# Attention and two feed-forward layers in one kernel: rows of x as dm = 96r + 32k + p, and the state updated head by head in 64-column tiles

## What is computed

```python
B, H, S, D = q.shape                      # 4, 8, 768, 48
f = 1.0 / (1.0 + np.exp(-f_logit))
for t in range(S):
    state = f[:, :, t, :, None] * state + np.einsum('bhd,bhe->bhde', k[:, :, t], v[:, :, t])
    y[:, :, t] = np.einsum('bhd,bhde->bhe', q[:, :, t], state)
x = y.transpose(0, 2, 1, 3).reshape(B * S, H * D)       # 3072 x 384
h = x @ w_in; x2 = (h * sigmoid(1.702 * h)) @ w_out     # 384 -> 2048 -> 384
p = probs / (probs.sum(-1) + 1e-9)
out = sum(p[:, e] * (relu(x2 @ w1[e]) @ w2[e]) for e in range(4))   # 384 -> 1024 -> 384
```

## Time and profile before

| | us |
|---|---|
| median of 3 runs (1355.3 to 1356.3) | 1356.08 |
| the profiled execution | 1355.08 |
| its span, first to last instruction | 1353.3 |
| PE busy | 1326.8 |
| DVE, POOL, ACT busy | 890.9, 629.0, 568.4 |
| half 0 alone | about 0 to 60 |
| seven rounds | about 60 to 536 |
| the rest | 536 to 1353 |

### The profile page before, as it was taken

The page is one execution under the profiler, slowest core; times in us unless marked ns, Lnnn a source line. Parts: engine busy times, 40 slices in busy tenths (PEclk is TensorE's granted clock), DMA queues, the critical chain, the costliest instruction groups (busy, mean ns, idle before and its releaser), DMA issues.

```text
span 1353.3 us, 26477 instructions
## 1 busy us (share of the span) xinstructions
PE 1326.8 (98%) x10837; PEld 1233.1 (91%) x10837; DVE 890.9 (66%) x1354; ACT 568.4 (42%) x975; POOL 629.0 (46%) x721
## 2 busy tenths in 40 slices
PE   6899999999999999999999999999999999999999
PEld 5788999999999999998999999999999999999998
DVE  8786858475858583566666666666666666666666
ACT  5673636363636363453233333333323433334341
POOL 8786747484747573655121212112212544443330
PEclk9999999999999999999999999999999999999999
DMA  9636252525252521220101101010001112222211
GB/s 157 135 74 104 60 84 63 86 61 85 62 88 59 87 59 40 79 74 24 35 13 35 36 13 35 12 36 24 25 24 59 36 47 70 71 70 75 66 35 47
DMA packets 240200, 79.34 MB, mean 59 GB/s; under 512 B 189136, under 2 KB 238544, under 8 KB 240080
## 3 DMA queue, kind: packets, MB, share of 16 engines
q1 hardware_dynamic: 201680, 74.11, 23.0%
q10 hardware_dynamic: 38400, 3.55, 2.2%
HBM read 67.83 MB, written 9.78 MB: 57 GB/s over the span
## 4 chain that ended last, share of the span: by engine, by line
PE 89%; ACT 3%; DVE 2%; issue 2%; POOL 2%; SPq 1%; DMA 1%; ACTq 0%; DVEq 0%; POOLq 0%
PE bank L1917 10%; PE bank L1915 10%; PE bank L1916 10%; PE bank L1851 9%; PE bank L1852 9%; PE bank L1850 9%; PE bank L1823 5%; PE bank L1582 4%; PE bank L1825 4%; PE bank L1824 4%; PE bank L1580 4%; PE bank L1581 4%; PE bank L1635 3%; PE bank L1591 1%; PE bank L1781 1%
## 5 line engine op out<-in xcount | busy, mean ns | idle before, releaser
L1529 DVE SCALAR_TENSOR_TENSOR acc<-bank,p_n,acc 128x384 f32<-128x384 f32 x384 | 235.0, 612 | 67.9 <-PE bank L1917 62.9
L1917 PE MATMUL bank<-w_h,h_l 128*128 128x384 f32 x768 | 257.3, 335 | 0.0
L1915 PE MATMUL bank<-w_h,h_h 128*128 128x384 f32 x768 | 257.2, 335 | 0.0
L1916 PE MATMUL bank<-w_l,h_h 128*128 128x384 f32 x768 | 257.0, 335 | 0.0
L1513 DVE TENSOR_TENSOR bank<-bank,x_copy 128x512 f32<-128x512 f32 x192 | 124.5, 694 | 165.9 <-ACT x_copy L1187 102.4
L836 POOL TENSOR_TENSOR g_l<-sig,g_h 128x384 fp32r<-128x384 f32 x128 | 157.7, 1232 | 157.4 <-ACT g_h L1090 157.3
L1852 PE MATMUL bank<-xs,we_l 128*128 128x512 f32 x528 | 206.5, 391 | 0.0
L1851 PE MATMUL bank<-xs,we_h 128*128 128x512 f32 x528 | 206.4, 391 | 0.0
L1850 PE MATMUL bank<-xs,we_h 128*128 128x512 f32 x528 | 205.5, 389 | 0.7 <-issue 0.7
L888 POOL TENSOR_TENSOR we_l<-we_raw,we_h 128x384 fp32r<-128x384 f32 x96 | 96.5, 1033 | 215.4 <-ACT we_h L1155 215.3
L1187 ACT ACTIVATE x_copy<-bank 128x512 f32<-128x512 f32 x144 | 86.1, 598 | 222.1 <-PE bank L1852 221.7
(11 more groups left out here) (156 smaller groups left out, 2387.2 us busy)
## 6 DMA issues: line engine op xcount, KB each, us to landing
we_raw<-in_moe_w SPq DMA_DIRECT2D x32, 384.0 KB, 3.9
w_raw<-in_moe_w SPq DMA_DIRECT2D x32, 384.0 KB, 3.3
v_sb<-in_v SPq DMA_DIRECT2D x48, 96.0 KB, 2.7
x_dram<-work SPq DMA_DIRECT2D x8, 576.0 KB, 4.7
x_raw<-x_dram SPq DMA_DIRECT2D x12, 384.0 KB, 4.4
f_raw<-in_f_logit SPq DMA_DIRECT2D x56, 72.0 KB, 2.1
q_raw<-in_q SPq DMA_DIRECT2D x56, 72.0 KB, 2.0
k_raw<-in_k SPq DMA_DIRECT2D x56, 72.0 KB, 2.1
```

The lines of the kernel that those rows point to most:

```text
L1529: dve.scalar_tensor_tensor(acc[:, pr * TT + i, :], y_bank[y % 3][:, 0:DM], p_n[:, col:col + 1], acc[:, pr * TT + i, :], ALU.mult, ALU.add) ...
L1915: pe.matmul(dst, hh, wh, start=f == 0, stop=False)
L1916: pe.matmul(dst, hh, wl, start=False, stop=False)
L1917: last = pe.matmul(dst, hl, wh, start=False, stop=f == 1)
```

## The change

x's rows in the three chunks of 128 become dm = 96r + 32k + p. v is laid out with 64 columns a head (48 and 16 zeros), and tile k of pair r takes 32 columns that stand side by side: k = 0 lies in the first head, k = 2 in the second, and k = 1 has 16 columns of each with zeros beside them, so it needs two products and the others one. `state_columns`, the transposes of half 0, VectorE's add into `y_rows` and the view of w_in follow the new order. The update of halves 1 to 7 becomes one product a head, 64 columns of `k_rows` by the head's 48 columns of v, at tile position (0, 0) or (0, 64).

```diff
-    VW = 3 * D
+    VW = 2 * GAP
-    win_v = w_in.rearrange("(p k) n -> k p n", p=P)
+    win_v = w_in.rearrange("(r k p) n -> k r p n", r=PAIRS, k=KT)
     def v_heads(c):
-        return v_sb[:, c, :, :].rearrange("p r (x d) -> p r x d", x=3)[:, :, 0::2, :]
+        return v_sb[:, c, :, :].rearrange("p r (j x) -> p r j x", j=2)[:, :, :, 0:D]
-    def v_columns(c, h, m):
-        lo = h % 2 * D + m
-        return v_sb[:, c, h // 2, lo:lo + 31 * KT + 1:KT]
+    TILE_PARTS = [(0, 0, 0), (1, 0, SQ), (1, 1, D), (2, 1, D + SQ)]
+    def v_columns(c, r, first):
+        return v_sb[:, c, r, first:first + SQ]
     def state_columns(r, m):
-        return state[:, r, m::KT]
+        return state[:, r, m * SQ:(m + 1) * SQ]
...
-            dve.memset(v_sb[:, :, :, D:2 * D], 0.0).then_inc(zeros_ready, 1)
+            dve.memset(v_sb[:, :, :, D:GAP], 0.0).then_inc(zeros_ready, 1)
...
-                    dve.tensor_tensor(y_rows[:, :], ring[u % 3][:, 0:DM], v_diag[:, :], ALU.add)\
+                    by_tile = y_rows[:, :].rearrange("p (k r x) -> p r k x", k=KT, r=PAIRS)
+                    dve.tensor_tensor(by_tile, ring[u % 3][:, 0:DM].rearrange("p (r k x) -> p r k x", k=KT, r=PAIRS),
+                                      v_diag[:, :].rearrange("p (r k x) -> p r k x", k=KT, r=PAIRS), ALU.add)\
...
-                for m in range(KT):
-                    for j in range(2):
-                        for r in range(PAIRS):
-                            last = add(r, m, v_columns(c, 2 * r + j, m), scores_T[:, c, 2 * r + j, :],
-                                       m == 0 and j == 0, m == KT - 1 and j == 1 and not from_state)
+                for m, j, first in TILE_PARTS:
+                    for r in range(PAIRS):
+                        last = add(r, m, v_columns(c, r, first), scores_T[:, c, 2 * r + j, :],
+                                   m == 0, m == KT - 1 and not from_state)
...
                     for r in range(PAIRS):
-                        into = ring[u % 3][0:GAP + D, r * 2 * D:(r + 1) * 2 * D].rearrange("p (j d) -> p j d", j=2)
-                        last = pe.matmul(into, k_rows[:, r * P:r * P + GAP + D], v_heads(c)[:, r, :, :],
-                                         start=True, stop=True)
+                        if fine(n):
+                            into = ring[u % 3][0:GAP + D, r * 2 * D:(r + 1) * 2 * D].rearrange("p (j d) -> p j d", j=2)
+                            last = pe.matmul(into, k_rows[:, r * P:r * P + GAP + D], v_heads(c)[:, r, :, :],
+                                             start=True, stop=True)
+                            continue
+                        for j in range(2):
+                            lo, h = GAP * j, 2 * r + j
+                            last = pe.matmul(ring[u % 3][lo:lo + GAP, h * D:(h + 1) * D],
+                                             k_rows[:, h * GAP:(h + 1) * GAP], v_head(c, h), start=True, stop=True,
+                                             tile_position=(0, lo))
...
-                        last = pe.transpose(ring[u % 3][:, m * P:(m + 1) * P], y_rows[:, m::KT], ident[:, :])
+                        last = pe.transpose(ring[u % 3][:, m * P:(m + 1) * P], y_rows[:, m * P:(m + 1) * P], ident[:, :])
```

More of the change, by code:

```diff
@@ L299, in v_heads @@
     def v_heads(c):
-        return v_sb[:, c, :, :].rearrange("p r (x d) -> p r x d", x=3)[:, :, 0::2, :]
+        return v_sb[:, c, :, :].rearrange("p r (j x) -> p r j x", j=2)[:, :, :, 0:D]
     def v_head(c, h):
-        lo = h % 2 * 2 * D
+        lo = h % 2 * GAP
         return v_sb[:, c, h // 2, lo:lo + D]
-    def v_columns(c, h, m):
-        lo = h % 2 * D + m
-        return v_sb[:, c, h // 2, lo:lo + 31 * KT + 1:KT]
+    TILE_PARTS = [(0, 0, 0), (1, 0, SQ), (1, 1, D), (2, 1, D + SQ)]
+    def v_columns(c, r, first):
+        return v_sb[:, c, r, first:first + SQ]
     def state_columns(r, m):
-        return state[:, r, m::KT]
+        return state[:, r, m * SQ:(m + 1) * SQ]
     def scores_of(i, L, n):
@@ L547, in load_v @@
                     for j in range(2):
-                        sp.dma_start(v_sb[:, c, :, 2 * j * D:(2 * j + 1) * D],
+                        sp.dma_start(v_sb[:, c, :, j * GAP:j * GAP + D],
                                      v_v[b, a, c, :, j::2, :]).then_inc(v_loaded, 16)
@@ L562, in load_piece @@
                 dst = stages[stage_of[i]][:, 0:width]
-                src = win_v[o // FF, :, o % FF:o % FF + width] if which == "in" else wout_v[:, o // DM, :]
+                src = win_v[o // FF, :, :, o % FF:o % FF + width] if which == "in" else wout_v[:, o // DM, :]
                 sp.dma_start(dst, src).then_inc(w_loaded[stage_of[i]], 16)
```

## The result

The changed kernel takes **1364.78 us** (median of 4 runs, 1364.01 to 1365.64), the kernel before 1356.19 us (4 runs, 1355.3 to 1356.7): a ratio of 1.0061, 95% interval 1.0045 to 1.0077. The forecast was 1346.7. The profiled execution took 1364.01 us, its span 1362.3 us, 9.0 more than before.

What follows compares the result with a forecast made beforehand. TensorE was taken to bound the kernel (busy 98% of the span). Savings of 9.2 us (y's tiles) and 3.2 (update), less 3.0 lost to waits, gave 9.4 us and a forecast of 1346.7 us, range 1342.5 to 1350.5.

Steps and rivals of the forecast that it cites:

- What bounds the kernel: Whole kernel: TensorE, busy 98% of the span; matmul time removed in the seven rounds comes off unless another engine is close.
- part 3: Everything outside y's products and the update's products: adds, v loads, y's add in half 0 and w_in's pieces, taken as 0.
- The rivals: Cheaper 48-column pace or free switch (0.19), other engines eat more (0.13), tile loads in turn (0.08), slower (0.04).
- the slower one: Update: two 64-column tiles don't run side by side, each product costs a full-array load; about 1366 us, chance 0.04.
- Part 1, y's tiles: y from v in later halves: 16 tiles instead of 24, 0.44 us saved in each of 21 chunks, 9.2 us.
- Part 2, the update: 17 of 20 updates: 8 products in two side-by-side tiles replace 4; 0.62 us instead of 0.81, 3.2 us saved.
- Where a part is lost: Rounds 1 and 3: y of chunk 2 waits for VectorE's state, in round 1 also line 1823 for GpSimd; 3.0 us lost.
- The sum: Whole kernel: 9.2 + 3.2 - 3.0 = 9.4 us saved, median 1346.7 us.

Runs made afterwards that it cites:

- flat_rows: The changed kernel, but w_in read through the view of the kernel before (one outer dimension of 128 rows): 1347.81 us, ratio 0.9934.
- before_outer4: The kernel before, with only w_in read as 4 outer groups of 32 rows: 1372.18 us (2 runs), ratio 1.0110.
- y_only: flat_rows with the old form of the update, so y's 16 side-by-side tiles without the tiled update: 1349.97 us, ratio 0.9948.
- update_only: The kernel before with only the update changed to one product a head in two 64-column tiles (halves 1 to 7): 1354.75 us, ratio 0.9979.
- by_pair_early_qk: The changed kernel with w_in in transfers of one pair's rows, and gates' loads and q and k quads issued ahead of later weight pieces: 1349.53 us, ratio 0.9946.

## Why the prediction was wrong, point by point

**What bounds the kernel** was right for the rounds and left out half 0. "What is taken from TensorE in these seven rounds comes off the time" held: about 10 us came off. But the change also touches six transfers ahead of the rounds, and no view of half 0 was read for them.

**The step that failed** stands in part 3: "The pieces of w_in come in as many rows of as many bytes: 0." Rows and bytes are indeed the same. What changed is the shape of the source, 4 x 32 rows instead of 128, and with it the number of DMA engines, 16 to 4. The term is not 0 but about 18 us: 12.7 to 12.9 us in half 0, the rest in round 1 (flat_rows against the change, 1347.81 and 1364.78, with kernels before that differ by 1.1 us: 18.1, and 17.2 between the profiled spans; before_outer4 against the kernel before: 14.9, and 16.4 between the spans). Two things should have stopped me. A term of zero wants the work that hides it named, and I named none; and v and the gates of half 1 stand behind w_in in the same queue, with ScalarE's wait for those gates down to 0.2 us before the change. Both were to be read in the profile. The number of engines was not: w_in's old form shows only 16. It needed the rule of the Trainium skill named above, which I had not brought to bear on this line.

**The rivals** had four mechanisms, all on TensorE or its partners in the rounds, and the slower one (column tiles not overlapping, 1366 us) came near the measured time for a wrong reason: its tiles do overlap (and its own terms, 20.6 less 9.2 us, give 1367.5). The range, 1342.5 to 1350.5, covered only uncertainty about terms that I had priced.

**Part 1, y's tiles**, was right. Foreseen: 672 instructions, about 11 us less busy time, 32 of them in 0.90 us. Seen: 672, 32.3 - 22.7 = 9.6 us less for TensorE and 26.9 - 17.1 = 9.8 for its loads, 0.90 us. Forecast 9.2 us, and 7.0 after the part lost to waits (2.2 of the 3.0 us); y_only gained 7.2.

**Part 2, the update**, was right in its size, and the row that it rests on was misread. Foreseen: 272 instructions, about 0.6 us to the next group. Seen: 272, 0.60. A pair of 64-column tiles side by side has (0.60 - 0.15) / 8 = 0.056 us, line 1601's price, not the 0.117 of a full load; the weight loads of the group are 9.3 / 272 = 0.034 us each. But line 1601's tiles do not stand side by side. Its `tile_position` is (lo, 0), with lo 0 or 64: they take turns between two groups of rows, in the same 64 columns. So the earlier trace rows said nothing of two tiles that use all rows, and that the new update has the same price, 0.028 us an instruction against the 0.029 forecast, is luck as far as that row goes; line 1591's column tiles, (0, lo), were the row that bore on it. Forecast 3.2 us, and 2.4 after waits (17 x 0.19 less 4 x 0.19); update_only gained 2.4. The Trainium skill's rule that I weighed there ("TensorE: Matmul & The Clock Gate", The mechanism: loads overlap only across row groups) does not hold for these column tiles: both use all rows. The same section also lets a load go ahead into a background weight buffer, which this case can't tell apart.

**Where a part is lost** was right in total and half right in its places. y of chunk 2 in round 1 of flat_rows:

```profile
124.81 0.68 DVE L1412 TENSOR_TENSOR state<-bank,state_faded 48x192 f32<-48x192 f32 x2
...
125.55 1.08 PE L1641 MATMUL bank<-scores_T,v_sb 128*32 128x128 f32 x32 [1.30 <-DVE state L1412]
...
129.91 0.44 PE L1836 MATMUL bank<-g_h,wout_h 128*128 128x384 f32 x1 [0.86 <-POOL g_l L840]
```

Against the earlier trace rows the wait for VectorE's state grows from 0.95 to 1.30 us, that for g_l from 0.42 to 0.86; in round 1. The forecast of "about 2.2 us in round 1" was too much, since VectorE's add came 0.8 us earlier as well (124.81 against 125.57): the moment that "doesn't move" did. In round 3 the forecast wait of 1.5 us isn't there at all, in flat_rows or in the change, and the 0.24 us of before is gone too; the round gains 1.5 us instead of 0.4. In return rounds 2, 5, 6 and 7, which the forecast held to be covered or free, gain 1.2, 1.4, 0.5 and 0.9 us in this trace and not 1.7 to 1.9. Round 6 has a wait of 0.93 us for VectorE's state. And a place that the forecast did not look at costs 0.4, 0.5 and 0.9 us in rounds 3, 5 and 7 of flat_rows, 0.4, 0.4 and 0.9 in the change: the first two slots of the round behind one that ends with an update of chunk 2, in round 7 with a wait of 0.39 us for VectorE's sig. The sum came out by offsetting errors: forecast 3.0 lost, and for flat_rows 21 x 0.45 + 17 x 0.21 = 13.0 gross against 9.5 measured by the medians, 3.5 lost, or 4.8 by the two spans.

**The sum.** Forecast -9.4 us; with the failed term taken out, flat_rows measures -9.5 (-7.1 to -11.0). The forecast was that of another kernel.

## What to carry to other kernels

When a change permutes rows, read the new access pattern of every transfer it touches, dimension by dimension: bytes and rows may stay the same while the slowest dimension, and with it the number of DMA engines, shrinks. A quick sign in a trace is a stretch in which the DMA share drops to 2 tenths while the issues on the queue grow from 0.4 to 2 us. And before an edit of an early transfer is put at zero, look at who stands behind it in the queue and how many tenths of a microsecond of slack that one has; splitting transfers mends the engines but lengthens the queue, so the late consumer's load has to move ahead as well.

## What the runs showed of the hardware

- A transfer of 128 rows of 2 KB went as if it used as many DMA engines as its slowest source dimension, up to 16 (busy shares of 2, about 5 and 9 tenths of the 16): 100 GB/s with 4, 200 with 8, 265 with 16, 385 where the rows were one dimension of 128. Transfers into 32 partitions each ran at 190 to 245 GB/s with all engines busy.
- Behind slow transfers, an issue of SyncE that takes 0.43 us took 2.42 us, without a semaphore to wait for, and the six issues of v took 10.75 us, not 5.01: slow transfers delay also the issue of the ones behind them that have other destinations.
- Two fp32 tiles of 64 columns side by side cost 0.056 us a pair of instructions with 48 moving columns, all rows in use.
- TensorE's granted clock was at its lower level from 37 to 49 us in the change, where TensorE had stood for 11.5 us, and from 88 to 94 us, after 3.3 us. In runs of one kernel (by_pair_early_qk) mean clocks of 0.999 and 0.995 went with 1346.5 to 1346.9 and 1351.3 to 1353.1 us. What lowered it in the slower of these runs is not shown.
